# First chunk's gate rows ahead of the others, g copied within SBUF, and the router's third tile as matrix products

## The chip, the core and the metric

One core of one Trainium2 chip runs the whole program. The metric is the device time of one execution in microseconds. The engines named below are PE (TensorE), DVE (VectorE), ACT (ScalarE), POOL (GpSimd) and SP (SyncE, which issues the bulk DMAs).

## The reference

Three layers follow one another. The first is a gated recurrence over 768 steps, for 2 batches of 8 heads of 40 features. With a running maximum m it keeps a 40x40 state C and a vector n:

```python
m_new = np.maximum(f_gate[:, :, t] + m, i_gate[:, :, t])
f_stab = np.exp(f_gate[:, :, t] + m - m_new)
i_stab = np.exp(i_gate[:, :, t] - m_new)
C = f_stab[:, :, None, None] * C + i_stab[:, :, None, None] * np.einsum('bhd,bhe->bhde', vt, kt)
n = f_stab[:, :, None] * n + i_stab[:, :, None] * kt
h_tilde = np.einsum('bhde,bhe->bhd', C, qt)
denom = np.maximum(np.abs(nq), 1.0)          # nq = n . q
y[:, :, t] = o * h_tilde / denom             # o = sigmoid(o_gate)
```

The result is 1536 tokens x 320. The second layer is a dense mixture of 4 experts (320 to 1024, relu, back to 320), weighted by given probabilities. The third chooses one of 8 experts for each token by the largest logit of `x @ w_gate`, gives each expert a capacity of 384 tokens in their order, and scales the result by the chosen probability.

## The kernel before

**Chunks and units.** The 768 steps are cut into 6 chunks of 128. A unit is one chunk of one batch (8 heads); the 12 units run in the order chunk by chunk, batch 0 then 1, so units 0 and 1 are the first chunk. Within a chunk the recurrence is a masked product: scores q.k times a decay matrix, times v. What came before the chunk enters through the state (`state`, 120 x 3 x 123, three groups of heads).

**Gate rows.** On 16 partitions (batch x head) DVE makes, over all 768 steps: `m_run` (scan), `decay`, `g_sum` (a scan of the log decays that restarts in each chunk), its split into two parts `g_split`, the bias rows `rows3[0:16]`, and the arguments `warg`, `garg`, `c_arg`; ACT takes their exponentials. `g_split` is written to DRAM (`g_saved_rows`) by SP and read back as two rows of `g_rows`; PE multiplies them by `spread_w`, which spreads g over 128 partitions and adds the causal mask (`spread_g`). PE transposes `rows3` chunk by chunk (`gate_columns`) and makes the carry factors `c_all`; DVE copies them into `cols3`, the per-step biases and weights.

**A unit** on PE (`attend`): scores (L469, 8 products), first half of `spread_g` for the next unit (L454), the part from before the chunk (L482), the update of the state (L490), the transpose of a finished tile (L508), then the sums with v (L500) in two halves, the second half of `spread_g` between them. ACT (`decays`, L752) makes the decay matrix of the next unit, POOL cuts its corner (`mask`, L926), weighs v (`weigh_v`, L936), scales the state (`carry_state`, L943), adds the new part (`new_state`, L952) and multiplies the output gate by the reciprocal of the denominator (`scale_o`, L964, result `osc`). DVE makes the product `pmat` (L1104), `before` (L1114), `state_new` (L1120), `total` (L1132), the denominator (L1140 to L1144) and `x_tok` (L1149).

**Order.** Each engine runs its own program, in the order in which it is written; they meet only at semaphores (`wait_ge`). `keep_warm` is products without use, to keep PE at work: 44 before the first transposes, 14 in two places. Each unit's data (q and k pairs, q rows, k and v) comes in four loads of SP into one of 4 buffers.

**First expert layer.** For each of 4 experts there are 4 blocks of 384 tokens. A block is `up` (8 tiles f of the hidden layer, 8 products each, L536 to L539) and `down` (3 tiles n of tokens, 24 products each, L551 to L553). ACT and DVE split the hidden tile in a high and a low part (L792, L1198). With the last expert (c = 0 to 3), the router runs beside it, one block behind: for the three tiles of the block before, DVE makes 24 dot products of a token tile with a gate column (`dots`, L1299), two after each of the 8 hidden tiles and 8 more at the end; then `choose_expert` gives `one_hot`, PE counts earlier tokens (`count_earlier`, L608, ahead of tile n = 2), and `gates_of` and `slots_of` give each token's gate and slot. The last group's logits are made on PE (`transpose_y`, L589, `logits`, L599).

## Time and profile before

| | |
|---|---|
| median of 3 runs | 608.98 us (607.63 to 617.74) |
| the profiled execution | 610.95 us |
| its span in the trace | 609.2 us |
| PE busy | 577.8 us, 95% |
| DVE busy | 318.7 us, 52% |
| ACT busy | 213.0 us, 35% |
| POOL busy | 204.2 us, 34% |
| mean granted clock of PE | 0.979 |

The span is what the trace covers; the execution's time is 1.75 us longer. Busy shares are means over a program of several stages; the chain of waits says which engine was last in each.

### The profile page before, as it was taken

Reading aid. Unit: us, or ns where it says so; the run is one execution under the profiler, and the core shown is the slowest. Engines: PE = TensorE matmul, PEld = TensorE weight load, DVE = VectorE, ACT = ScalarE, POOL = GpSimd, SP = SyncE. Lnnn points to the kernel's source line nnn. Section 1 sums busy time; section 2 is a strip of 40 time slices with the busy share of each in tenths; the row PEclk is TensorE's granted clock in tenths of the full one; section 3 lists DMA queues with packets and bytes.
Section 4 is the critical chain, followed back from the end, with each engine's and each line's share of the span. In section 5 each row is a group of like instructions: output and inputs, shape, how many; then the busy total and the mean of one; then the engine's idle time right before and its main releaser. Section 6 shows DMA issues by size and latency. Waiting matters only on the chain.

```text
span 609.2 us, 10906 instructions
## 1 busy us (share of the span) xinstructions
PE 577.8 (95%) x3924; PEld 566.5 (93%) x3924; DVE 318.7 (52%) x741; ACT 213.0 (35%) x457; POOL 204.2 (34%) x226
## 2 busy tenths in 40 slices
PE   3999999999999999999999999999879998899996
PEld 3899989999999999999999999898868998899996
DVE  8389883322332332233233237797844499855472
ACT  5455572311321231232133023023115386546341
POOL 6266556101100110110111022223132467765461
PEclk9699999999999999999999999999987999899999
DMA  6486707941101101110110110111133657764400
GB/s 200 114 261 182 225 30 268 366 179 47 47 1 47 47 0 47 47 46 2 47 47 0 47 48 10 66 61 41 48 122 112 206 182 247 244 223 140 139 16 18
DMA packets 22574, 64.32 MB, mean 106 GB/s; under 512 B 3206, under 2 KB 12559, under 8 KB 22412
## 3 DMA queue, kind: packets, MB, share of 16 engines
q1 hardware_dynamic: 20620, 59.80, 30.0%
q0 software_dynamic: 1920, 4.07, 1.8%
q8 instruction: 21, 0.34, 0.2%
q14 instruction: 13, 0.11, 0.1%
HBM read 52.98 MB, written 13.11 MB: 108 GB/s over the span
## 4 chain that ended last, share of the span: by engine, by line
PE 79%; DVE 10%; ACT 3%; DMA 3%; issue 2%; POOL 2%; POOLq 0%; SPq 0%; DVEq 0%; ACTq 0%
PE bank L536 26%; PE bank L551 8%; PE bank L553 8%; PE bank L552 8%; DVE products L1299 5%; PE bank L539 4%; PE bank L538 4%; PE bank L683 3%; PE bank L682 3%; PE bank L500 3%; PE bank L681 3%; PE bank L469 2%; PE bank L454 1%; PE bank L482 1%; DVE h_lo L1198 1%
## 5 line engine op out<-in xcount | busy, mean ns | idle before, releaser
L792 ACT ACTIVATE h_hi<-bank 128x384 fp32r<-128x384 f32 x192 | 94.5, 492 | 300.6 <-PE bank L539 299.5
L1198 DVE SCALAR_TENSOR_TENSOR h_lo<-bank,h_hi 128x384 fp32r<-128x384 f32 x192 | 105.8, 556 | 111.5 <-ACT h_hi L792 110.6
L906 POOL TENSOR_TENSOR w_lo_odd<-stage,w_hi_odd 128x512 fp32r<-128x512 f32 x24 | 31.3, 1302 | 149.0 <-DVE w_hi_odd L1163 119.7
L906 POOL TENSOR_TENSOR w_lo_even<-stage,w_hi_even 128x512 fp32r<-128x512 f32 x24 | 32.2, 1344 | 118.0 <-DVE w_hi_even L1163 104.8
L536 PE MATMUL bank<-xt_hi,w_hi_even 128*128 (+2 forms) x192 | 65.3, 340 | 3.8 <-DVE h_lo L1198 2.1
L536 PE MATMUL bank<-xt_hi,w_hi_odd 128*128 128x384 f32 (+2 forms) x192 | 62.9, 327 | 2.7 <-DVE h_lo L1198 2.3
L536 PE MATMUL bank<-xt_lo,w_hi_even 128*128 (+2 forms) x192 | 63.7, 332 | 0.0
L536 PE MATMUL bank<-xt_hi,w_lo_even 128*128 (+2 forms) x192 | 63.6, 331 | 0.0
L1207 DVE SCALAR_TENSOR_TENSOR acc<-bank,prob,acc 128x320 f32 (+1 forms) x36 | 19.6, 551 | 80.9 <-PE bank L553 79.8
L536 PE MATMUL bank<-xt_lo,w_hi_odd 128*128 128x384 f32 (+2 forms) x192 | 61.8, 322 | 0.0
L536 PE MATMUL bank<-xt_hi,w_lo_odd 128*128 128x384 f32 (+2 forms) x192 | 61.8, 322 | 0.0
L551 PE MATMUL bank<-w_hi_odd,h_hi 128*128 128x320 f32 x192 | 60.2, 313 | 1.3 <-DVE h_lo L1198 1.3
L551 PE MATMUL bank<-w_hi_even,h_hi 128*128 128x320 f32 x192 | 59.4, 310 | 0.1
L552 PE MATMUL bank<-w_lo_odd,h_hi 128*128 128x320 f32 x192 | 59.4, 309 | 0.0
L553 PE MATMUL bank<-w_hi_even,h_lo 128*128 128x320 f32 x192 | 59.4, 309 | 0.0
L553 PE MATMUL bank<-w_hi_odd,h_lo 128*128 128x320 f32 x192 | 59.3, 309 | 0.0
L552 PE MATMUL bank<-w_lo_even,h_hi 128*128 128x320 f32 x192 | 59.3, 309 | 0.0
L536 PEld LDWEIGHTS bank<-xt_hi,w_hi_even 128*128 128x128 f32 x192 | 36.9, 192 | 4.8 <-DVE h_lo L1198 2.6
L536 PEld LDWEIGHTS bank<-xt_hi,w_hi_odd 128*128 128x128 f32 x192 | 36.1, 188 | 4.2 <-DVE h_lo L1198 4.2
L1299 DVE SCALAR_TENSOR_TENSOR products<-acc,wg_rows 128x320 f32<-128x320 f32 x72 | 38.6, 582 | 0.1
L551 PEld LDWEIGHTS bank<-w_hi_odd,h_hi 128*128 128x128 f32 x192 | 36.1, 188 | 2.1 <-DVE h_lo L1198 2.1
L536 PEld LDWEIGHTS bank<-xt_lo,w_hi_even 128*128 128x128 f32 x192 | 36.9, 192 | 0.0
(187 smaller groups left out, 1347.5 us busy)
## 6 DMA issues: line engine op xcount, KB each, us to landing
stage<-w_moe SPq DMA_DIRECT2D x48, 704.0 KB, 4.1
slot_rows<-empty_row SPq DMA_DIRECT2D x1, 4632.0 KB, 22.8
x_slot<-slot_rows SPq DMA_DIRECT2D x24, 193.0 KB, 4.4
kv<-kv_tok SPq DMA_DIRECT2D x12, 324.0 KB
qk_pair<-qk_pair_t SPq DMA_DIRECT2D x24, 160.0 KB
q_rows<-q_t SPq DMA_DIRECT2D x12, 180.0 KB
sig<-o_tok SPq DMA_DIRECT2D x2, 960.0 KB, 6.3
out<-empty_row SPq DMA_DIRECT2D x2, 960.0 KB, 18.8
```

Of the source, the lines that this page charges most:

```text
L500: mm = pe.matmul(ps_in[:, h * V1:(h + 1) * V1], pmat[:, h, :], v41[j][:, h, :], start=True, stop=True)
L536: pe.matmul(dst, wk[w][:, k, cols], xk(k), start=(n == 0), stop=False)
L538: pe.matmul(dst, w1_hi[w][:, 2, cols], xh(2), start=False, stop=False)
L539: pe.matmul(dst, w1_hi[w][:, 2, cols], xl(2), start=False, stop=True).then_inc(h_psum, 1)
L551: pe.matmul(ps_y[n][:, 0:X], h_hi[:, f, rows], w2_hi[w][:, f, :], start=(f == 0), stop=False)
L552: pe.matmul(ps_y[n][:, 0:X], h_hi[:, f, rows], w2_lo[w][:, f, :], start=False, stop=False)
L553: mm = pe.matmul(ps_y[n][:, 0:X], h_lo[:, f, rows], w2_hi[w][:, f, :], start=False, stop=(f == FT - 1))
L792: act.activation(h_hi[:, f, :], ps_h[f % 3][:, 0:BLOCK], ACT.Relu).then_inc(h_hi_done, 1)
L906: return pool.tensor_tensor(w1_lo[w][:, :, cols], raw1[:, 0:2, :], w1_hi[w][:, 0:2, cols].bitcast(F32), ALU.subtract)
L1198: dve.scalar_tensor_tensor(h_lo[:, f, :], ps_h[f % 3][:, 0:BLOCK], 0.0, h_hi[:, f, :].bitcast(F32), ALU.max, ALU.subtract).then_inc(h_done, 1)
L1207: op = dve.scalar_tensor_tensor(acc[:, tile, 0:X], ps_y[n][:, 0:X], share, acc[:, tile, 0:X], ALU.mult, ALU.add)
L1299: dve.scalar_tensor_tensor(products[k % 3][:], acc[:, t, 0:X], 1.0, wg_rows[:, n % E2, :], ALU.mult, ALU.mult, accum_out=logit[:, t, n % E ...
```

## The change

**Gate rows in two parts.** DVE first makes all rows of chunk 0 (128 steps), then those of the other five. The bias rows of the later chunks come after unit 0, their `garg` and `warg` are made on POOL, their columns are transposed after units 0 and 1 have begun (`bias_columns`, `other_columns`).
**g.** `g_split` is copied straight to `g_rows` within SBUF, one DMA for each of its two parts (two a unit); the DRAM copy is gone. The mask of the second `g_rows` buffer is copied by ACT from the first instead of being made on POOL.
**ACT.** A sigmoid of one column comes first; both large sigmoids stay ahead of the first exp, of 16x128 instead of 16x768; those of the later chunks come after both units' decays.
**No state work in units 0 and 1.** No product with the empty state, no `before`, no `carry_state` and `new_state`; the update is written straight into the state.
**PE.** 110 `keep_warm` products from the moment `ones` is set; then the scores of unit 0 before its first `spread_g`; 24 in unit 0, 12 in unit 1.
**POOL.** `scale_o` of the unit before comes ahead of `weigh_v` and `carry_state`, not behind them.
**Loads.** q rows, k and v are one array, padded to 128 rows; q and k pairs are padded to 48 rows: three loads a unit. SP's loop over units is written out. The first piece of the weights is loaded after all units' data, with the others. `probs` is loaded later and normalised on DVE after the loop of units.
**Router.** Dots for two of three tiles: those of a block's first tile in the same block's `down` phase, those of the second one by one in the next `up` phase. The third tile's logits are made on PE in that phase (transposes ahead of f = 1, products ahead of f = 2). `count_earlier` moves ahead of n = 1, f = 4.

```diff
-    WARM_SHORT, WARM_GAP, WARM_LONG = 44, 14, 34
+    DOT_TILES = 2
+    PE_TILES = [NT * c + DOT_TILES for c in range(BLOCKS1 - 1)] + list(range(TILES - NT, TILES))
+    WARM_SHORT, WARM_GAP, WARM_LONG = 110, (24, 12), 34
...
-                sp.dma_start(q_rows[j][:], q_t[u]).then_inc(unit_in[j], 16)
-                sp.dma_start(kv[j][:], kv_tok[u]).then_inc(unit_in[j], 16)
+                    sp.dma_start(qk_pair[j][s * HALF:s * HALF + QK], qk_pair_t[u, s]).then_inc(unit_in[j], 16)
...
-                sp.dma_start(g_rows[b][0:2].bitcast(F32), g_dram[:, b * HEADS:(b + 1) * HEADS, bass.ts(c, P)]).then_inc(g_in[b], 16)
+                for n in range(2):
+                    sp.dma_start(g_rows[b][n:n + 1].bitcast(F32), g_split[b * HEADS:(b + 1) * HEADS, n, c * P:(c + 1) * P].bitcast(F32)).then_inc(g_in[b], 16)
...
+            load_unit(0, 0)
+            sp.wait_ge(mask_rows, BATCHES)
+            sp.wait_ge(g_lo_done, 1)
+            for b in range(BATCHES):
+                load_g(0, b)
+            load_unit(0, 1)
+            load_unit(0, 2)
+            sp.wait_ge(g_lo_done, 2)
+            sp.wait_ge(g_spread, 2)
+            load_g(1, 0)
+            load_unit(0, 3)
+            sp.wait_ge(g_spread, 4)
+            load_g(1, 1)
             sp.dma_start(prob[:], probs).then_inc(small_in, 16)
             sp.dma_start(wg[:], w_gate).then_inc(small_in, 16)
-            load_unit(0, 0)
...
+            def first_columns():
+                pe.wait_ge(gate_exp, 1)
+                pe.transpose(ps_upd[:, 0:80], rows3[:, 0:P], ident[0:80, 0:80]).then_inc(cols_pe, 1)
...
+            def bias_columns():
+                pe.wait_ge(gate_step, GATE_BIAS)
...
+            def other_columns():
+                pe.wait_ge(gate_exp, 3)
...
+            def attend(i, r, last_chunk=False, opening=None):
...
+                if opening is None:
+                    scores(i, r)
+                if not last and opening != 1:
                     spread_g(i, r + 1, 0)
-                pe.wait_ge(state_done, u + 1)
...
+                if opening == 1:
+                    scores(i, r)
+                    carry_columns()
+                if opening == 1:
+                    pe.wait_ge(state_done, 1)
+                if opening is None:
+                    pe.wait_ge(state_done, u - EMPTY + 1)
...
+                if opening is not None:
+                    keep_warm(WARM_GAP[opening], ones[:], ones[:])
+                if opening == 1:
+                    bias_columns()
...
+            pe.wait_ge(pool_const, CONST_ONES)
+            keep_warm(WARM_SHORT, ones[:], ones[:])
+            pe.wait_ge(pool_const, CONST_SPREAD)
+            scores(0, 0)
             spread_g(0, 0, 0)
+            first_columns()
             spread_g(0, 0, 1)
-            keep_warm(WARM_GAP, ones[:], tri[:])
-            gate_columns()
-            attend(0, 0, warm=WARM_GAP)
-            attend(0, 1)
+            attend(0, 0, opening=0)
...
+                    if c and f == 2:
+                        logits(PE_TILES[c - 1])
+                    if c and f == 1:
+                        transpose_y(PE_TILES[c - 1])
                 def before_products(n, f):
-                    if c and n == 2 and f == 0:
+                    if c and n == 1 and f == 4:
...
+            act.wait_ge(mask_rows, 1)
+            act.activation(g_rows[1][:], g_rows[0][:].bitcast(F32), ACT.Copy).then_inc(mask_rows, 1)
...
-            act.wait_ge(gate_step, GATE_ROWS)
-            act.activation(rows3[32:48, :], warg[:], ACT.Exp).then_inc(gate_exp, 1)
-            act.activation(rows3[64:80, :], garg[:], ACT.Exp).then_inc(gate_exp, 1)
-            act.activation(c_scale[:], c_arg[:], ACT.Exp).then_inc(gate_exp, 1)
+            act.wait_ge(gate_step, GATE_COLS)
+            act.activation(rows3[32:48, 0:P], warg[:, 0:P], ACT.Exp).then_inc(gate_exp, 1)
...
+            act.wait_ge(gate_step, GATE_C)
+            act.activation(c_scale[:], c_arg[:], ACT.Exp).then_inc(carry_exp, 1)
+            act.wait_ge(warg_done, 1)
+            for to, argument in ((32, warg), (64, garg)):
+                act.activation(rows3[to:to + BH, P:], argument[:, P:], ACT.Exp).then_inc(gate_exp, 1)
+            act.wait_ge(bias_done, 1)
...
+            pool.wait_ge(cols_done, 1)
+            weigh_v(0)
+            mask(0)
+            pool.wait_ge(gate_step, GATE_G)
+            pool.tensor_tensor(later_chunks, g_sum[:, later].rearrange("h (c t) -> h c t", t=P),
+                               d_start[:, 1:].unsqueeze(2).broadcast_to([BH, CHUNKS - 1, P]), ALU.add)
+            weigh_v(1)
+            mask(1)
+            pool.wait_ge(gate_step, GATE_BIAS)
+            pool.tensor_tensor(warg[:, later].rearrange("h (c t) -> h c t", t=P), rows3[0:BH, later].rearrange("h (c t) -> h c t", t=P),
+                               g_sum[:].rearrange("h (c t) -> h c t", t=P)[:, 1:, P - 1:P].broadcast_to([BH, CHUNKS - 1, P]),
+                               ALU.add).then_inc(warg_done, 1)
+            for u in range(1, UNITS - BATCHES):
+                scale_o(u - 1)
                 if u + 1 < UNITS - BATCHES:
+                    if u == 1:
+                        pool.wait_ge(cols_done, 2)
+                        pool.wait_ge(carry_done, 1)
                     weigh_v(u + 1)
                     carry_state(u + 1)
-                if u:
-                    scale_o(u - 1)
                 mask(u + 1)
-                new_state(u)
+                if u >= EMPTY:
+                    new_state(u)
...
+            running_max(early)
+            decay_rows(early)
+            chain(dve.tensor_tensor_scan(g_sum[:, 1:P], reset[:, 1:P], decay[:, 1:P], 0.0, ALU.mult, ALU.add))
+            g_parts(early)
+            chain(dve.tensor_tensor(rows3[0:BH, early], gate_i[:, early], m_run[:, 1:P + 1], ALU.subtract))
+            bias_rows(early)
+            chain(dve.tensor_tensor(warg[:, early], rows3[0:BH, early], g_sum[:, P - 1:P].broadcast_to([BH, P]), ALU.add))
+            assert done[0] == GATE_COLS
+            running_max(later)
+            decay_rows(later)
+            chain(dve.tensor_tensor(rows3[0:BH, later], gate_i[:, later], m_run[:, P + 1:S + 1], ALU.subtract))
+            assert done[0] == GATE_ROWS
+            dve.wait_ge(cols_pe, 1)
+            dve.tensor_copy(cols3[:, 0, :], ps_upd[:, 0:80]).then_inc(cols_done, 1)
             chain(dve.tensor_copy(d_start[:].unsqueeze(2), chunks(decay[:])[:, :, 0:1]))
+            chain(dve.memset(chunks(decay[:])[:, 1:, 0:1], 0.0))
+            chain(dve.tensor_tensor_scan(g_sum[:, later], reset[:, later], decay[:, later], 0.0, ALU.mult, ALU.add))
+            assert done[0] == GATE_G
+            chain(dve.tensor_tensor(c_arg[:].unsqueeze(2), chunks(g_sum[:])[:, :, P - 1:P], d_start[:].unsqueeze(2), ALU.add))
+            assert done[0] == GATE_C
...
+            g_parts(later)
+            dve.wait_ge(pool_const, CONSTS)
+            probabilities(0, 0)
+            combine(0, 0)
+            bias_rows(later)
+            assert done[0] == GATE_BIAS
+            probabilities(0, 1)
+            dve.wait_ge(carry_pe, 1)
+            dve.wait_ge(bias_pe, 1)
+            dve.tensor_copy(c_all[:].rearrange("p n c -> p (n c)"), ps_first[0:GR, 0:BATCHES * 3 * CHUNKS]).then_inc(carry_done, 1)
+            dve.tensor_copy(cols3[:, 1:, 0:BH], ps_first[:, P + BH:P + CHUNKS * BH].rearrange("p (c g) -> p c g", g=BH)).then_inc(bias_done, 1)
+            combine(0, 1)
+            dve.wait_ge(cols_pe, 2)
+            dve.tensor_copy(cols3[:, 1:, 2 * BH:], ps_t[:, 80:CHUNKS * 80].rearrange("p (c g) -> p c g", g=80)[:, :, 2 * BH:]).then_inc(cols_done, 1)
+            dve.wait_ge(cols_done, 2)
+            with dve.Fori(0, UNITS // 4 - 1) as i:
+                for r in range(2, 6):
+                    attend(i, r)
...
+                    dve.wait_ge(log_ready, group + 1)
+                    log = ps_log(t.start, t.stop)
                     if group < LAST1:
-                        dve.wait_ge(dot_done, NT * E2 * (group + 1))
+                        t2 = PE_TILES[group]
                         log = logit[:, t, :]
-                    else:
-                        dve.wait_ge(log_ready, group - LAST1 + 1)
...
+            def dots(t, experts):
+                dve.wait_ge(y_free, 3 + 3 * (G1 - BLOCKS1) + t + 1)
+                for one in experts:
+                    k = DOTS * (t // NT) + t % NT * E2 + one
                     if k >= 3:
                         dve.wait_ge(dot_done, k - 2)
-                    dve.scalar_tensor_tensor(products[k % 3][:], acc[:, t, 0:X], 1.0, wg_rows[:, n % E2, :], ALU.mult, ALU.mult,
-                                             accum_out=logit[:, t, n % E2:n % E2 + 1]).then_inc(dot_done, 1)
...
                     if c:
-                        dots(c - 1, f)
+                        dots(NT * (c - 1) + 1, [f])
...
+                    if c < LAST1 and n < 2:
+                        dots(NT * c, range(n * E2 // 2, (n + 1) * E2 // 2))
```

The places where order matters. PE, from its start to the first sums of unit 0, before (`rows` is `rows3`):

```order
L415 MATMUL bank<-tri,ones 128x128 x43
L437 MATMUL bank<-ident,rows 128x16 x5
L454 MATMUL bank<-g_rows,spread_w 128x512 [waits g_in0]
L454 MATMUL bank<-g_rows,spread_w 128x512
L415 MATMUL bank<-tri,ones 128x128 x14
L421 MATMUL bank<-ident,rows 128x80 [waits gate_exp]
L425 MATMUL bank<-c_scale,c_select 120x6 [waits select_done]
L469 MATMUL bank<-qk_pair 128x128 [waits unit_in0]
L415 MATMUL bank<-tri,ones 128x128 x14
L454 MATMUL bank<-g_rows,spread_w 128x512 [waits exp_done,cols_done,g_in1]
L482 MATMUL bank<-state,q_rows 128x123 [waits comb_done,state_done]
L500 MATMUL bank<-kv,pmat 128x41 [waits p_done]
```

and with the change:

```order
L426 MATMUL bank<-ones 128x128 x109
L482 MATMUL bank<-qk_pair 128x128 [waits unit_in0,pool_const]
L471 MATMUL bank<-g_rows,spread_w 128x512 [waits g_in0]
L431 MATMUL bank<-ident,rows 128x80 [waits gate_exp]
L471 MATMUL bank<-g_rows,spread_w 128x512
L471 MATMUL bank<-g_rows,spread_w 128x512 [waits g_in1]
L516 MATMUL bank<-vw,kvq 120x123 [waits vw_done]
L426 MATMUL bank<-ones 128x128 x24
L530 MATMUL bank<-kvq,pmat 128x41 [waits p_done]
```

The scores of unit 0 and its first spread now stand ahead of any transposed column, a single transpose stands ahead of the first sums instead of twelve and the carry products, and the product with `state` is gone.

DVE, from the gates' arrival to the first `pmat`, before:

```order
L1066 SCALAR_TENSOR_TENSOR m_run<-gate_f,gate_i 16x768 [waits gates_in]
L1067 TENSOR_TENSOR decay<-gate_f,m_run 16x768 [waits gate_step]
L1068 TENSOR_TENSOR decay<-decay,m_run 16x768 [waits gate_step]
L1071 SCALAR_TENSOR_TENSOR g_sum<-reset,decay 16x768 [waits gate_step]
L1072 CAST g_split<-g_sum 16x768 [waits gate_step]
L1074 TENSOR_TENSOR g_split<-g_sum,g_split 16x768 [waits gate_step]
L1078 TENSOR_TENSOR rows<-decay,g_sum 16x768 [waits pool_const,gate_step]
L1082 TENSOR_TENSOR gate_f<-rows,g_sum 16x768 [waits gate_step]
L1083 TENSOR_TENSOR gate_i<-g_sum,d_start 16x768
L1089 COPY cols<-bank 128x6x48 [waits gate_pe]
L1091 COPY c_all<-bank 120x36 [waits gate_pe]
L1104 TENSOR_TENSOR pmat<-bank,dmat 128x4x128 [waits s_ready,masked,y_free]
```

and with the change:

```order
L1128 SCALAR_TENSOR_TENSOR m_run<-gate_f,gate_i 16x128 [waits gates_in,gate_step]
L1156 SCALAR_TENSOR_TENSOR g_sum<-reset,decay 16x127 [waits gate_step]
L1137 CAST g_split<-g_sum 16x128 [waits gate_step]
L1138 TENSOR_TENSOR g_split<-g_sum,g_split 16x128 [waits gate_step]
L1160 TENSOR_TENSOR gate_f<-rows,g_sum 16x128 [waits gate_step]
L1128 SCALAR_TENSOR_TENSOR m_run<-gate_f,m_run,gate_i 16x640 [waits gate_step]
L1130 TENSOR_TENSOR decay<-gate_f,m_run 16x640 [waits gate_step]
L1165 TENSOR_TENSOR rows<-gate_i,m_run 16x640 [waits gate_step]
L1168 COPY cols<-bank 128x80 [waits cols_pe,gate_step]
L1171 SCALAR_TENSOR_TENSOR g_sum<-reset,decay 16x640 [waits gate_step]
L1137 CAST g_split<-g_sum 16x640 [waits gate_step]
L1186 TENSOR_TENSOR pmat<-bank,dmat 128x4x128 [waits s_ready,masked,pool_const]
```

The split of g for chunk 0 (`g_split` 16x128) now comes fourth and fifth here; the scan and split of the other chunks stand between the first columns and the first `pmat`.

POOL in the loop of units, one unit, before:

```order
L936 TENSOR_TENSOR vw<-kv,cols 128x328 [waits upd_ready,unit_in3]
L943 TENSOR_TENSOR state_kept<-state,c_all 120x369 [waits state_done]
L964 TENSOR_TENSOR osc<-sig,rden 128x320 [waits x_main,rden_done]
L926 AFFINE_SELECT dmat<-dmat 2x8x2 [waits exp_done]
L952 TENSOR_TENSOR state<-state_new,state_kept 120x369 [waits state_step,state_carried]
```

and with the change:

```order
L1010 TENSOR_TENSOR osc<-sig,rden 128x320 [waits x_main,rden_done,sig_done]
L986 TENSOR_TENSOR vw<-kvq,cols 128x328 [waits upd_ready,unit_in0]
L993 TENSOR_TENSOR state_kept<-state,c_all 120x369 [waits state_done]
L976 AFFINE_SELECT dmat<-dmat 2x8x2 [waits exp_done]
L1002 TENSOR_TENSOR state<-state_new,state_kept 120x369 [waits state_step,state_carried]
```

`osc` (scale_o) moved from behind `vw` and `state_kept` to ahead of them; both now follow its wait for `rden_done`.

## Rows read from the trace of the kernel before

**Rows 1.** The chain that ended last, first 60 us, in order of time: start, us, what.

```profile
3.24 1.76 DVE m_run L1066
...
5.02 0.96 DVE decay L1067
...
6.98 0.19 DVE d_start L1069
...
12.33 2.23 DMA g_saved_rows<-g_split
...
14.57 1.71 DMA g_rows<-g_saved_rows
...
19.28 2.50 PE bank L425 x12
21.77 2.01 PE bank L469 x16
...
34.84 1.09 PE bank L469 x16
...
36.99 0.67 PE bank L490 x6
37.66 0.33 PE bank L508 x3
37.99 0.82 PE bank L500 x8
...
39.93 1.09 PE bank L469 x16
```
**Rows 2.** A window of 1 us on PE: length, busy time, granted clock, DMA share, GB/s.

```profile
26.00:27.00 1.00, 1.00 (x7) 0.50 0.00 0
```
**Rows 3.** Timeline of all engines, first 20 us: start, us, engine, line, operation.

```profile
5.04 1.08 POOL L885 TENSOR_SCALAR_AFFINE_SELECT spread_w<-spread_w 128x128 fp32r<-128x128 f32 x1
...
9.39 4.82 PE L415 MATMUL bank<-tri,ones 128*128 128x128 bf16 x44 [9.39 <-DVE g_sum L1071]
9.69 1.81 ACT L735 ACTIVATE sig<-sig 128x1920 f32<-128x1920 f32 x1 [0.98 <-DMA sig<-o_tok]
...
11.51 1.28 ACT L737 ACT_TABLE_LOAD   x1
...
16.22 0.84 ACT L737 ACTIVATE rows<-gate_f 16x768 f32<-16x768 f32 x1 [3.43 <-DVE c_arg L1084]
...
18.07 2.09 ACT L752 ACTIVATE dmat<-bank,cols 128x128 f32<-128x128 f32 x8
```
**Rows 4.** Timeline of all engines, 20 to 42 us.

```profile
23.91 1.29 DVE L1104 TENSOR_TENSOR pmat<-bank,dmat 128x512 f32<-128x512 f32 x2 [0.27 <-PE bank L469]
...
37.11 0.79 POOL L943 TENSOR_TENSOR state_kept<-state,c_all 120x369 f32<-120x369 f32 x1
37.17 0.76 DVE L1140 SCALAR_TENSOR_TENSOR den<-total 128x8 f32<-128x8 f32 x1
...
38.45 0.72 POOL L964 TENSOR_TENSOR osc<-sig,rden 128x320 f32<-128x320 f32 x1 [0.56 <-DVE rden L1144]
...
40.46 0.23 POOL L926 TENSOR_SCALAR_AFFINE_SELECT dmat<-dmat 2x16 f32<-2x16 f32 x1 [1.28 <-ACT dmat L752]
```
**Rows 5.** The chain again, starts of three blocks of the first expert layer.

```profile
346.37 1.04 PE bank L536 x6
...
368.02 1.04 PE bank L536 x6
...
392.14 1.04 PE bank L536 x6
```
**Rows 6.** Timeline of PE where it waits for the router's choice.

```profile
388.29 0.17 PE L608 MATMUL bank<-one_hot,tri 128*128 128x24 bf16 x1 [1.06 <-DVE one_hot L1252]
```
**Rows 7.** Timeline of PE, the router's logit products of one tile.

```profile
440.75 0.82 PE L599 MATMUL bank<-wg,yT 128*128 128x8 f32 x6
```
**Rows 8.** The page's costliest groups, the router's dot products.

```profile
L1299 DVE SCALAR_TENSOR_TENSOR products<-acc,wg_rows 128x320 f32<-128x320 f32 x72 | 38.6, 582 | 0.1
```

319 lines of the change are left out of this document (156 added, 163 removed).

## The prediction

> **What bounds the kernel now.** I read the page first: PE is busy 95% of the span, so outside a few places only less PE work could help. The chain of waits shows those places. Until 18 us it holds almost no matmul: it is the gate rows on DVE (a scan of 16x768, 1.76 us, two additions of 0.96), then g to DRAM (2.23) and back (1.71) [rows 1]. Then it is all PE, but at half pace: the scores of unit 0 take 2.01 us, those of unit 2, 1.09 [rows 1], and the granted clock still stands at 0.50, the 1.2 GHz level, at 26 [rows 2]. Unit 2 begins at 34.84, unit 3 at 39.93: a unit costs 5.09 us, all on PE [rows 1]. The third place is the last layer of the first expert set. A block begins at 346.37, the next at 368.02: 21.65 us with nothing to wait for. The next takes 24.12 (to 392.14) [rows 5], because DVE is behind with the router's dots and PE waits for its choice [rows 6].
>
> **The opening, step by step.** My ruler is when unit 3 begins on PE, 39.93 now; what follows is paced by PE at 5.09 a unit.
>
> DVE. A fixed part of about 0.15 us (the 16x6 copy took 0.19) plus length: 16x128 costs about 0.42 as scan and 0.28 as addition, 16x640 1.5 and 0.82, a tile 328 to 369 wide 0.5 [rows 1]. The early chain is two scans, two additions, the split of g (two operations), two additions for the bias and one for warg: 3.24 + 1.85 + 0.3, so g of chunk 0 is ready at about 5.4 instead of 12.3, and the early arguments at about 6.3.
>
> The copy of g. One DMA step instead of two removes about 2.2 [rows 1]. But it is queued behind both o_gate halves and unit 0, 2.9 MB; I expect it to land at 11.5 to 12.5, so of the 6.9 us that DVE gains here only some 4 count.
>
> ACT. It must still do both sigmoids before the first exp: the second starts at 9.69 and takes 1.81, then the table load 11.51 + 1.28 = 12.79 [rows 3]. The new dummy sigmoid only takes a table load out of ACT's idle time. The mask copy (128x1024, about 1 us by the sigmoid's 1.81 for 1920 [rows 3]) lies in the idle time ahead of the first sigmoid, which waits for its data: free, unless the mask is late, when it delays the sigmoids by as much. Exp of 16x128 is about 0.3 (16x768: 0.84 [rows 3]): 13.1. Transpose and copy: 13.7. Eight exps, 2.1 to 2.3 [rows 3]: unit 0's decays are complete at 16.0, its mask at 16.2. So ACT, not g, is what the first unit now follows.
>
> DVE again. After the copy at 13.7 it does d_start, the scan of 16x640, c_arg and the split of later g: 0.2 + 0.1 + 1.5 + 0.2 + 1.7 gives 17.4; POOL's garg, 1.4 us by POOL's 369-wide product of 0.79 [rows 4], can lock it out in this stretch, so I take 17.9. Here DVE, not ACT, is late. Product of unit 0 (1.29 [rows 4]) to 19.2, against 25.2 now. Then the state copy, 0.5, while PE does the sums (two times 0.82 in the chain, the second half after the product, with a spread of g [rows 1]), and the copy of the total, 0.5: 20.6; bias rows 0.8: 21.4; product of unit 1 to 22.7. Then it waits for PE: scores 1.1, carry columns 1.25, upd 0.67, twelve warming products 0.65, five small transposes 0.45 at full clock, from 20.2: 24.3. At half clock the same is 2.0 + 2.5 + 1.3 + 1.3 + 0.9, that is 28.2 (2.01 and 2.50 are shown, 1.09 and 0.67 too [rows 1]; the warming by 109 ns each [rows 3]; the rest halved or doubled).
>
> From there, full clock: two copies 0.5, denominator 0.7, state copy 0.5, x of unit 0 behind POOL's scale_o 1.3, total 0.4, last columns 0.4: 28.1 with no overlap, 27.6 with. POOL follows with weigh_v 0.73, carry_state 0.79 and the mask 0.23: 29.4. Product of unit 2 to 30.7, PE's second half 0.7: unit 3 begins at 31.4. Gain 8.5 us at full clock throughout; at half clock the step above costs 3.9: 4.6. Left out of units 0 and 1 are six products of state and the adding; they lie in this sum as zero, since PE is no longer what is last there.
>
> **Which clock.** The 44 warming products before took 4.82 us, 109 ns each [rows 3], and 16 units of scores half as long at 34.84 as at 21.77. So PE ran at the low level at first, whatever the page grants there; the clock rose, fell after PE had little to do between 14.2, when the products end, and 16.3, when g landed, and was low at 26 still, through small transposes and 6-column products. Afterwards PE starts at 1.1 instead of 9.4: 110 products end between 9 (clock up early) and 13 (never up), and scores wait for unit 0 at about 11.5. There will be a hole of up to 2.5 us and again small work. I take two chances in three that part of the opening runs low, and the middle: 6.5 us. The Trainium skill (TensorE: Matmul & The Clock Gate, What's actually happening) says the low clock is the default and activity releases it; by that alone the long run of products would leave the opening at full clock, 8.5 us. The rows of before, where 4.8 us of products did not carry through, speak for less.
>
> **The loop of units.** POOL now does scale_o(u-1) ahead of weigh_v and carry_state. In unit 2 osc starts at 38.45, since it waits for the reciprocals; 0.72 and then two products of at most 0.79 and the mask's 0.23 end at 40.98; today the mask ends at 40.69 [rows 4]. But the product of unit 3 also needs unit 3's scores, which end at 39.93 + 1.09 = 41.02 [rows 1]. It just fits. The denominator, 0.76 us beside POOL's carry_state [rows 4], can only get quicker; x's product may get slower. Zero, bounds -0.5 and +2. The normalising of probs, four small operations, 1.4 us, moves from a hole into the last pass of DVE: 0 to 0.7. Piece 0 of the weights is now loaded with the other three, behind all units; those are not waited for today, and all four are 2.9 MB, under 10 us at the rate at which the first 2.9 MB came (by 12 us): hidden. The unit's loads are 3 instead of 4 and 9% larger; hidden.
>
> **The router.** Per block PE loses 24.12 - 21.65 = 2.47 us [rows 5]. A third of the dots (24 of 72, 38.6 / 72 = 0.54 us each [rows 8]) leaves DVE and another third moves into the down phase before; DVE's choice comes about 2.7 us after the up phase, PE asks for it 5.3 after. So the waits go. PE gets three transposes, 0.33 [rows 1], and a tile's logit products, 0.75 of the 0.82 shown [rows 7], and keeps the count, 0.2: 1.3 us. Gain 1.15 in two blocks; the last gains 1.3, as a wait of 0.5 for the slots of the earlier group stays. Sum 3.6, bounds 2.5 and 4.5.
>
> **Sum.** 6.5 + 3.6 = 10.1 us. The profiled execution took 610.95: 600.9. The median of the runs is 2.0 lower, 608.98: I forecast **599**, 1.6% faster. 2%, about what a measurement of this kernel can tell from no change, would be 596.8.
>
> **Rivals.** (a) *Clock up and short waits*: full gain of 8.5 or a little more, with 3.6 to 4.5: 594.5 to 596.8. For it: DVE's later work may not meet POOL's. Chance 0.25. (b) *Half clock through both first units*: 4.6 or less, 601 to 603. For it: PE's work there is small transposes and products. Chance 0.16. (c) *The change doesn't shorten the opening*: the copy of g is stuck behind the bulk loads, or the mask copy pushes the sigmoids back; unit 0 starts at 16 rather than 13.7, and only 3 to 4 of the opening's gain with the router's remain: 602 to 605. Against it: the queue was nearly empty at 12 us. Chance 0.05. (d) *Slower, by POOL and DVE shutting each other out in the loop*. A POOL select started beside a DVE addition took 1.08, ending with it [rows 1, 3]. If scale_o, weigh_v, carry_state and the mask were each held up so, by some 0.8 us of an addition's 0.96, a unit would take 5.09 + 3.2; over 9 units +29, 628. It makes the kernel slower than before from 10 / 9 = 1.1 us a unit on, by over 2% from 2.5. Against it: the same POOL operations took 0.72 and 0.79 beside DVE work [rows 4]. Chance 0.03. The Trainium skill (SBUF — State Buffer, the section on the engine and DMA ports) has this as a lock held for a whole instruction, between POOL and a DVE operation that reads two SBUF inputs. By that rule x's product (total times osc) would wait for all of weigh_v, 0.7 us; I have this as absorbed by the slack behind the total.
>
> **How the numbers follow.** Forecast, part of the opening at low clock: 597 to 601, chance 0.51. With (a) to (d) that is one. The range leaves out (d) and the far ends of (a) and (c): 594.5 to 604. Faster by over 2%: (a), 0.25. Within 2%: 0.72. Slower: (d), 0.03.
>
> **What would show it.** Right: g_rows lands near 12, first decay near 13.7, product of unit 0 near 18, unit 3's scores at 31 to 35, units at 5.09; blocks of the router at 22.9. Wrong: PE waiting for POOL in the loop; first exp after 14; unit 3 after 36; PE waiting for transposes of the third tile.

## The result and the profile after

The changed kernel took 616.6 us (median of 4, 611.3 to 618.9), the kernel before 609.8 beside it: ratio 1.0124, 95% interval 1.0069 to 1.0179. A second series, 12 runs of the changed kernel beside 17 of the kernel before on one chip, gave 614.5 against 610.7, ratio 1.0070 (1.0026 to 1.0114). A ratio compares the runs within 1.5% of the fastest of their kernel; medians and ranges are of all runs. So it is slower by about 1%, within 2% of the kernel before, and 599 with the range to 604 was wrong. The profiled execution below took 611.34, the shortest of the four (span 609.6, mean granted clock 0.971; the other three 0.957 to 0.963; before: 610.95, 609.2, 0.979).

The chain that ended last, of the changed kernel, in order of time (start, us, what), answers to [rows 1] and [rows 5]:

```profile
4.11 10.00 DMA kvq<-kvq_tok
...
14.24 2.08 PE bank L482 x16
...
17.28 0.24 DVE cols L1168
...
17.75 1.95 DVE g_sum L1171
...
20.63 1.48 issue
22.11 0.68 DVE pmat L1186
...
30.73 3.57 PE bank L530 x16
...
36.04 2.01 PE bank L482 x16
...
43.63 1.09 PE bank L482 x16
...
48.72 1.09 PE bank L482 x16
```
```profile
350.86 1.04 PE bank L572 x6
...
372.50 1.04 PE bank L572 x6
...
395.53 1.04 PE bank L572 x6
...
418.62 1.04 PE bank L572 x6
```

Unit 3 began at 43.63, where [rows 1] has 39.93 and I expected 31.4 to 35.3. Until 14.11 the chain is no longer gate rows but unit 0's own load; from 17.28 to 22.11 it lies on DVE; most of units 1 and 2 runs at half pace (scores of unit 2: 2.01). From 43.63 a unit takes 5.09, as before. The router's blocks start 21.64, 23.03 and 23.09 apart, where [rows 5] has 21.65 and 24.12. Added up from the two profiled executions: 3.7 us lost at unit 3, 0.9 more by the first expert's products (below), 2.9 gained in the router's blocks; that leaves 1.6 at 460 us, of which the last layers give back 1.2.

The clock of TensorE, windows of the two kernels (from:to, length, busy us and count of PE, PEld, DVE, ACT, POOL, granted clock, DMA share, GB/s). Before:

```profile
17.70:27.90 10.20, 10.11 (x65) 9.33 (x64) 3.82 (x9) 3.57 (x14) 3.18 (x5) 0.51 0.51 135
28.00:60.00 32.00, 32.00 (x309) 30.40 (x307) 26.52 (x59) 17.20 (x60) 20.09 (x30) 1.00 0.72 210
```

After:

```profile
0.00:14.00 14.00, 7.59 (x110) 7.42 (x110) 8.55 (x18) 8.78 (x13) 5.00 (x17) 1.00 0.84 245
14.10:20.90 6.80, 6.37 (x37) 5.22 (x38) 3.42 (x7) 3.20 (x12) 1.83 (x3) 0.50 0.85 208
20.90:27.70 6.80, 5.76 (x63) 5.35 (x61) 5.48 (x8) 1.21 (x5) 3.36 (x4) 1.00 0.43 123
27.80:41.40 13.60, 13.60 (x76) 12.37 (x76) 4.87 (x16) 4.91 (x15) 3.76 (x6) 0.50 0.46 124
41.50:60.00 18.50, 18.50 (x183) 17.53 (x181) 15.56 (x34) 10.55 (x36) 12.07 (x18) 1.00 0.60 167
```

The last figure but two of a row is the granted clock: 0.50 is the 1.2 GHz level. (The 1.00 of the first row is too high for its beginning: until 3.86 the warming products took 0.103 us each, 27 in 2.79, and from 3.9 on 0.055, 86 in 4.70.) Before, the low level lasted 10.2 us and was over when unit 1 began. After, it is there for 6.8 us behind a hole of 5.6, gives way for 6.8, and comes back for 13.6, in which PE has no idle time at all: from 27.8 to 41.4 units 1 and 2 are worked at half speed. What stands at the holes, by the timelines of DVE, POOL and PE (start, us, engine, line, operation, idle time before it and what ended it):

```profile
5.75 2.86 SPq L347 DMA_DIRECT2D g_rows<-g_split  x4
...
13.45 0.31 ACT L784 ACTIVATE rows<-gate_f 16x128 f32<-16x128 f32 x1
```
```profile
14.24 2.08 PE L482 MATMUL bank<-qk_pair 40*128 40x128 f32 x16 [5.58 <-DMA kvq<-kvq_tok]
...
22.84 1.08 PE L530 MATMUL bank<-kvq,pmat 128*128 128x41 f32 x8 [1.04 <-DVE pmat L1186]
```
```profile
20.43 1.75 DVE L1138 TENSOR_TENSOR g_split<-g_sum,g_split 16x640 fp32r<-16x640 f32 x1
```
```profile
20.03 1.47 POOL L1020 TENSOR_TENSOR reset<-g_sum,d_start 16x640 f32<-16x640 f32 x1
```

The four copies of g took 0.71 us each to issue on the mean, where a read of g from DRAM before took 0.24 to 0.27; unit 0's data came at 14.11, 0.7 us behind the start of the first exponential; the difference for the later g stood beside POOL's sum, 1.75 instead of the 0.81 it takes alone (below). The normalising of the probabilities now stands in DVE's last pass, and PE waits for it:

```profile
79.71 0.21 DVE psum_p L1285
...
79.94 1.06 DVE psum_p L1287
...
82.35 1.09 PE bank L530 x8
```

### The profile page after: what moved, and what is told of

The parts are those of the page before. It is cut to its first block, busy times and chain, and to the rows that moved or that the text cites. A ratio compares the mean times of both kernels' runs of the same rounds, so it can differ in the third digit from the quotient of the medians.

```text
span 609.6 us, 10961 instructions
## 1 busy us (share of the span) xinstructions
PE 585.8 (96%) x4012; PEld 575.4 (94%) x4012; DVE 306.0 (50%) x702; ACT 214.2 (35%) x465; POOL 200.4 (33%) x221
## 4 chain that ended last, share of the span: by engine, by line
PE 88%; DVE 3%; issue 3%; DMA 3%; ACT 2%; POOL 1%; SPq 1%; POOLq 0%; DVEq 0%; ACTq 0%
PE bank L572 29%; PE bank L587 9%; PE bank L589 9%; PE bank L588 9%; PE bank L575 5%; PE bank L574 5%; PE bank L530 3%; PE bank L727 3%; PE bank L726 3%; PE bank L725 3%; PE bank L482 2%; DMA kvq<-kvq_tok 2%; PE bank L471 1%; PE bank L516 1%; PE bank L508 1%
## 5 line engine op out<-in xcount | busy, mean ns | idle before, releaser
L797 ACT ACTIVATE dmat<-bank,cols 128x128 f32<-128x128 f32 x96 | 27.1, 371 | 29.5 <-PE bank L471 25.7
L572 PEld LDWEIGHTS bank<-xt_hi,w_lo_even 128*128 128x128 f32 x192 | 36.4, 190 | 0.0
```

What stands on the lines that cost most here:

```text
L572: pe.matmul(dst, wk[w][:, k, cols], xk(k), start=(n == 0), stop=False)
L797: op = act.activation(dmat[b][:, h, :], src[:, n * P:(n + 1) * P], ACT.Exp, bias=cols3[:, c, b * HEADS + h:b * HEADS + h + 1])
```

## The experiments

The first run takes half of the change alone. (A span or a mean clock without another name is that of a kernel's profiled execution; medians are of all timed runs.)

**The router alone** (lines of the diff on tiles, dots, transposes, logits and their waits, on the kernel before).

> The kernel before with the router's part of the change alone: six of an expert's dot products of the first two tiles stay on VectorE, the third tile's go to TensorE, and nothing of the opening, the loads or the loop of units is touched. If the blocks of the router gain what the profile of the changed kernel shows (block starts 21.64, 23.03 and 23.09 apart where two of them were 24.12 and 24.18, and the last stretch 0.74 shorter), the run ends 2.9 us below the kernel before, about 607, and the whole loss of the changed kernel stems from its opening. Rival: the router's gain is given back in the stages behind it (its blocks end earlier, but the clock falls for longer there), and this run ends level with the kernel before, within 1 us.

608.6 against 610.9, ratio 0.9955 (0.9917 to 0.9993). The router gains about 2.7 us (0.4 to 5.1 by the interval) and keeps them.

**All but the router.**

> The changed kernel with the router of before: the other half of the change, its opening, loads and loop of units, alone. If the two halves add up, it ends some 3 us above the changed kernel, 619 to 620, or 10 us above the kernel before. Rival: the two halves meet in some other way (the shifted times of the blocks alone bring the clock's falls), and this run is level with the kernel before or with the changed kernel.

616.4, ratio 1.0118 (1.0057 to 1.0180). Some 7 us of loss, where the changed kernel has 4 to 7 with the router's gain in it; by the number it is the rival, level with the changed kernel (616.6) and not the 619 to 620 that the halves add up to, though the intervals don't tell the two apart. The loss is there without the router, and not with the router alone: it is that of the opening, the loads and the loop.

**More products ahead of unit 0.**

```diff
-    WARM_SHORT, WARM_GAP, WARM_LONG = 110, (24, 12), 34
+    WARM_SHORT, WARM_GAP, WARM_LONG = 220, (24, 12), 34
```

> The changed kernel with 220 warming products ahead of unit 0 instead of 110, so that TensorE has no hole of 5.6 us between 8.66 and 14.24. Nothing else is altered, and the data of unit 0 still land at 14.1. Theory of the clock: the fall to 0.50 at 14.2 and what follows it come from the hole, so the clock stays at 1.00 past 14; then unit 3 starts some 4 to 6 us sooner than 43.6, and the run ends 4 to 8 us below the changed kernel, near 610. Rival one: the products of units 0 to 2 wait for data and for VectorE and leave holes of their own, so the clock falls anyway a few us later, and the run gains under 2 us. Rival two: 220 products take longer than until 14.1 (at 0.05 each they end near 14.2) and push unit 0, a loss of up to 1 us.

617.4, ratio 1.0097 (1.0051 to 1.0143): nothing gained. The windows:

```profile
0.00:25.20 25.20, 20.93 (x289) 19.89 (x289) 14.83 (x28) 12.71 (x28) 8.70 (x21) 1.00 0.78 195
25.40:52.50 27.10, 27.10 (x150) 25.13 (x151) 11.57 (x29) 8.20 (x27) 7.74 (x12) 0.50 0.50 135
```

and the timeline of PE:

```profile
15.57 1.31 PE L482 MATMUL bank<-qk_pair 40*128 40x128 f32 x16 [0.29 <-DMA kvq<-kvq_tok]
...
23.04 1.09 PE L530 MATMUL bank<-kvq,pmat 128*128 128x41 f32 x8 [2.20 <-DVE pmat L1186]
...
38.37 2.08 PE L482 MATMUL bank<-qk_pair 40*128 40x128 f32 x16
...
47.94 2.08 PE L482 MATMUL bank<-qk_pair 40*128 40x128 f32 x16
```

The first theory was right up to 14 us and wrong behind: the clock held past unit 0, PE then waited 2.20 us for DVE's product, and 2.4 us later came 27 us of the low level. Units 2 and 3 are 9.57 us apart there, against 5.09: each unit at the low level costs 4.5 us. This is rival one.

**Units 1 and 2 asked for later.**

```diff
             for b in range(BATCHES):
                 load_g(0, b)
+            sp.wait_ge(unit_in[0], UNIT_LOADS)
             load_unit(0, 1)
```

> The changed kernel with one wait more in the load queue: units 1 and 2 are asked for only when unit 0 has landed, so that they no longer share the DMA engines with it. Theory of the data: unit 0's load took 10.0 us since units 1 and 2 ran beside it; alone it lands near 11.5, the hole on TensorE is 2.8 us instead of 5.6, and the first product of probabilities comes no sooner than ACT's first exponential at 13.5 allows; unit 3 starts 2 to 3 us sooner and the run ends 2 to 4 us below the changed kernel, unless unit 1's data, then some 3 us later than now, become the wait (TensorE asks for them at about 26, far behind). Rival: unit 0 lands at 14 all the same, since the output gates' 960 KB and not the later units' data hold the engines; then nothing moves, within 1 us.

```profile
13.66 2.08 PE L483 MATMUL bank<-qk_pair 40*128 40x128 f32 x16 [4.84 <-DMA kvq<-kvq_tok]
```

```profile
11.00:12.00 1.00, 0.00 (x0) 0.00 (x0) 0.00 (x0) 0.98 (x2) 0.00 (x0) 0.50 0.80 287
12.00:12.80 0.80, 0.00 (x0) 0.00 (x0) 0.00 (x0) 0.80 (x1) 0.00 (x0) 0.50 0.06 13
12.80:13.50 0.70, 0.00 (x0) 0.00 (x0) 0.00 (x0) 0.32 (x2) 0.00 (x0) 0.50 0.00 0
```

Unit 0 began at 13.7, and between 13.5 and 15.6 in seven profiled executions of kernels that left those two loads where they were. It lies among them, so no effect of the later units shows; the rival holds: with them out of the way the data came no sooner. Its reason holds only in part. In the run further on with unit 0 ahead of the second half of the gates it landed at 10.1 (issued at 3.11, 7.0 to landing), so its place in the queue counts. But here the DMA engines had all but stopped by 12 and moved nothing from 12.8 to 13.5 (the last two figures of a row), and the load was counted as landed at 13.53 only. What that last microsecond is, no run shows. Its four runs (604.3 to 626.4, clocks 0.941 to 0.982) are too far apart for a ratio; no gain is to be seen.

**DVE in another order:** the scan and split of the later rows ahead of the first columns' copy.

```diff
-            dve.wait_ge(cols_pe, 1)
-            dve.tensor_copy(cols3[:, 0, :], ps_upd[:, 0:80]).then_inc(cols_done, 1)
...
             g_parts(later)
+            dve.wait_ge(cols_pe, 1)
+            dve.tensor_copy(cols3[:, 0, :], ps_upd[:, 0:80]).then_inc(cols_done, 1)
```

> The changed kernel, in which VectorE does the scan of the 640 later rows and its split into two halves ahead of the copy of the first columns, in the hole where it waited from 10.6 to 17.3 for TensorE's transpose. Nothing is left out. Theory of the order on VectorE: in the changed kernel the scan (1.95), its small copies, the cast (0.49) and the difference (1.75, beside GpSimd's sum) stood between the first columns at 17.3 and unit 0's first product with the scores at 22.1; they leave that chain, so that product comes when the mask does, at about 20.3, some 1.8 us sooner, TensorE's hole of 1.04 at 21.8 goes, and the run ends 2 us below the changed kernel where the clock stays as it is, and more where fewer holes keep the clock up (mean granted clock above 0.963). Rival: the clock's fall is not decided by that hole, and the mean clock stays near 0.963; then 0 to 2 us below the changed kernel, about 615.

> The same order on VectorE, and 220 warming products ahead of unit 0, which end with the landing of its data at 14 to 15.3, so that both holes of TensorE's (5.6 us and 1.0 to 2.2 us) are gone. Theory of the holes: with neither hole the clock stays at 1.00 through units 0 and 1, the low stretch of 13.7 to 27.3 us at the loop's entry is not there, the mean clock is at 0.98 or above, and the run ends near 602, 8 us below the kernel before. Rival: the clock falls all the same once the units' small products begin, whatever stands ahead of them, and the run ends at 612 to 617 with a mean clock under 0.97, as with the 220 products alone.

The first, with 110 warming products, took 611.3, ratio 1.0002 (0.9948 to 1.0057), the second, with 220, 609.8, ratio 1.0040 (1.0003 to 1.0076). The order alone brings the changed kernel level with the kernel before, more than the 2 us expected; the second is not the 602 expected, and below its rival's 612 to 617. The timeline of DVE in the second:

```profile
10.96 1.48 DVE L1169 TENSOR_TENSOR_SCAN g_sum<-reset,decay 16x640 f32<-16x640 f32 x1
...
13.17 0.81 DVE L1138 TENSOR_TENSOR g_split<-g_sum,g_split 16x640 fp32r<-16x640 f32 x1
18.00 0.24 DVE L1266 COPY cols<-bank 128x80 f32<-128x80 f32 x1 [4.01 <-PE bank L431]
20.86 1.29 DVE L1184 TENSOR_TENSOR pmat<-bank,dmat 128x512 f32<-128x512 f32 x2 [2.62 <-POOL dmat L976]
```

The product comes 2.9 us behind the columns and no longer 4.8, as forecast, and the split alone takes 0.81. In both profiled executions the low level still came at 31, for 24 us, without a hole above 0.7 us behind the first unit's scores. These two executions were the longest of their kernels (622.2 and 621.8, mean clocks 0.947 and 0.954), so they show that such a fall occurs, and not that it is usual. The strong form of my theory, no hole and no fall, is refuted all the same; the median clock of the runs was 0.966 and 0.976, where the changed kernel has 0.963 over all its 16 runs and the kernel before 0.979.

**Both gaps filled** (220 and 60 products), then **the second alone** (110 and 60).

```diff
-    WARM_SHORT, WARM_GAP, WARM_LONG = 110, (24, 12), 34
+    WARM_SHORT, WARM_GAP, WARM_LONG = 220, (60, 12), 34
```

> The changed kernel with 220 warming products ahead of unit 0 and 60 instead of 24 behind its sums for the state. With the 220 alone the clock held to 25 us and then stood at 0.50 for 27.3 us; the one long hole before the fall was 2.2 us at 20.8. Here it is filled with 36 products of 0.06 us, at no cost while the clock is up. Theory of the holes: the low stretch of 27 us goes, and the run ends some 8 to 12 us below 617, near 606. Rival: the fall comes without the hole, at about the same time; then the run ends at 617 or above it, up to 2 us more since the added products take 0.107 each at the low clock.

> The changed kernel with 60 instead of 24 warming products behind unit 0's sums, and its 110 ahead of unit 0 as they were: the gap of 1.0 to 2.2 us at 21 is filled, that of 5.6 us ahead of unit 0 stays. With both filled the run took 607.9, with the first alone 617.4. If the fall at 14 costs only its own stretch and the second gap is what throws the loop's entry into the low clock, this run ends at 609 to 612, near the one with both filled. Rival: the first hole has already brought the clock down when the 36 added products come, they take 0.107 each (3.9 us, of which 1.0 us in the gap), and what follows is low all the same: 617 to 620.

Both: 607.9, ratio 0.9995 (0.9948 to 1.0042), median clock 0.979. The second alone: 615.0, ratio 1.0125 (1.0072 to 1.0179), median clock 0.964. With the first alone at 1.0097 and neither at 1.0070 to 1.0124, it takes both in most runs. It does not in each: the eight runs with the second alone lie from 605.2 to 618.7, too far apart for their ratio to carry much, seven of them with mean clocks of 0.959 to 0.971, like the changed kernel's (614.5 beside them). The eighth, its profiled execution, took 605.2 at 0.981: the hole ahead of unit 0 was 6.6 us there, the clock low for 10.2 us across it, and back at 1.00 from 21 to 440. The kernel with both lost its clock elsewhere in the profiled execution; its timeline of PE and windows:

```profile
37.31 1.16 PE L482 MATMUL bank<-qk_pair 40*128 40x128 f32 x16
...
76.11 1.08 PE L530 MATMUL bank<-kvq,pmat 128*128 128x41 f32 x8 [0.61 <-DVE pmat L1186]
```
```profile
0.00:78.40 78.40, 75.17 (x834) 71.09 (x836) 58.92 (x132) 42.71 (x130) 40.36 (x66) 1.00 0.72 207
78.80:88.80 10.00, 10.00 (x50) 9.68 (x47) 7.59 (x19) 6.86 (x13) 4.12 (x5) 0.51 0.00 0
```

Unit 3 at 37.31, with the clock at 1.00 all the way there, and a fall 2 us behind the wait for the probabilities.

**Dense products at the loop's entry** (`keep_warm(48, ones[:], ones[:])` behind the last spread before the loop).

> The changed kernel with 48 dense products more between unit 1 and the loop of units; the holes of the opening are all there. They cost 2.7 us at full clock and 5.1 us at half. Theory that the loop's own products are what keeps the clock low once it is entered low (the changed kernel stood at 0.50 for 13.7 us with TensorE without a hole): dense products at its entry bring the clock back before the loop, the low stretch from 27.7 is 6.8 to 10.2 us, and the mean clock rises from 0.963 to 0.97 or more; the run ends level with the changed kernel or up to 3 us below. Rival: what the clock does there depends on the opening's holes alone and not on what stands at the loop's entry; then the products' own time comes on top, 3 to 5 us above the changed kernel, at 620.

619.0, ratio 1.0153 (1.0055 to 1.0251), with 17 us of the low level at 25.6 in its profiled execution, across the added products: the rival. Here they only took time.

**The normalising back in a hole** (with the load of the probabilities right behind unit 0's), on the kernel with both gaps filled, and **all edits together**: new order, normalising, 205 and 32 products.

```diff
             assert done[0] == GATE_ROWS
+            dve.wait_ge(small_in, 32)
+            dve.tensor_reduce(psum_p[:], prob[:], AX_X, ALU.add).then_inc(prob_step, 1)
...
             with dve.Fori(0, UNITS // 4 - 1) as i:
                 for r in range(2, 6):
                     attend(i, r)
-            dve.wait_ge(small_in, 32)
-            dve.tensor_reduce(psum_p[:], prob[:], AX_X, ALU.add).then_inc(prob_step, 1)
```

> The kernel with both gaps filled (220 and 60 warming products), and the normalising of the probabilities moved from the end of the loop of units to VectorE's hole ahead of the first columns. In the run with the gaps filled TensorE waited 0.61 us for it at 75.5, and 2 us behind that the clock stood at 0.50 for 10.2 us; so did it behind the same wait in three other runs. Theory: that wait brings that fall; without it no low stretch stands between 40 and 440, and the run ends 0.8 us of path and up to 5 us of clock below the 607.9 of the kernel with the gaps filled, at 603 to 605. Rival: the fall at 78 comes of something else at the end of the units (their last products wait for nothing else, but the experts' first do, by 0.4 us); it is still there, and the run ends within 1 us of 607.9.

> The changed kernel with four edits at once: the scan of the later rows and its split ahead of the first columns on VectorE, the normalising of the probabilities there too instead of at the end of the loop of units (their load goes into the queue behind unit 0's), 205 warming products ahead of unit 0 and 32 behind its sums. By the theory of the holes none of TensorE's waits before the experts is left but a short one for GpSimd at 19, so the clock stays at 1.00 from the start to the router: unit 3 starts near 35.5 (39.9 before, 43.6 in the changed kernel, 37.3 with the gaps filled alone), the router gives its 2.9, the mean clock is 0.985, and the run ends at 601 to 603, 7 us below the kernel before. Rival: the clock's fall at the loop's entry comes now and then whatever stands ahead of it, and the mean of the runs stays at 0.975 or below and their median within 2 us of the kernel before.

The first: 606.9, ratio 0.9939 (0.9896 to 0.9983), median clock 0.987. It has no low stretch between 40 and 440, but one of 10 us at 29 in the profiled execution. Against 603 to 605 expected, the median is 1.0 below the 607.9 of both gaps filled, which is the rival's bound; against the kernel before beside each it is 0.6% lower, with intervals that overlap. So a gain is likely and its size open. All edits: 606.5, ratio 0.9950 (0.9897 to 1.0003), where 601 to 603 was expected. Its profiled execution (604.6) has the clock at 1.00 throughout the opening, and unit 3 where I expected it for this run (35.5), but 4.5 us behind the 31.4 of the prediction's full-clock sum. Unit 0 begins at 15.47 and not at 11.5: its data landed at 14.1 (issued at 3.89, 10.2 to landing), and the 205 warming products, at 15.5, end later still:

```profile
15.47 1.16 PE L482 MATMUL bank<-qk_pair 40*128 40x128 f32 x16
...
22.97 1.16 PE L482 MATMUL bank<-qk_pair 40*128 40x128 f32 x16
...
30.15 1.16 PE L482 MATMUL bank<-qk_pair 40*128 40x128 f32 x16
...
35.95 1.16 PE L482 MATMUL bank<-qk_pair 40*128 40x128 f32 x16
```
```profile
0.00:440.00 440.00, 434.69 (x3095) 428.17 (x3095) 207.15 (x504) 138.38 (x321) 113.88 (x139) 1.00 0.29 92
```

In the twelve runs the clock was 0.987 or 0.988 in six (601.8 to 604.6) and 0.968 to 0.976 in six (608.5 to 613.5): with the holes gone low runs are fewer than in the changed kernel, where all 16 are at 0.971 or below, but not gone. The rival (mean 0.975 or below, within 2 us of the kernel before) isn't met either: the mean is 0.980, the median 4.8 below.

**Unit 0's load between the output gates' halves**, on the kernel with all edits.

> The first kernel of this batch (all four edits) with unit 0's load put between the two halves of the output gates instead of behind both. Unit 0 then lands near 11 instead of 14 to 15, but the second half of the gates some 3 us later, and ACT does its sigmoid ahead of the first exponential. Theory: the opening is bound twice, by unit 0's data and by ACT's two sigmoids, and the second takes the first's place: the first columns come at 16 to 17.5 as now, and the run ends within 1.5 us of the kernel with the four edits. Rival: data alone were the bound; the first product with the probabilities comes 2 to 3 us sooner, and so does the end.

608.5, ratio 0.9965 (0.9923 to 1.0007). The timeline of ACT:

```profile
15.28 1.80 ACT L783 ACTIVATE sig<-sig 128x1920 f32<-128x1920 f32 x1 [6.12 <-DMA sig<-o_tok]
...
18.39 0.31 ACT L785 ACTIVATE rows<-gate_f 16x128 f32<-16x128 f32 x1
```

PE had its scores at 13.9 and then waited 3.3 us for this exponential, 4.9 later than in the changed kernel. The opening is bound twice, as expected; the columns came later than expected, though, behind 18.39, and the median is 2.0 above the kernel with all edits, where at most 1.5 was expected.

**The old opening, warm, with the new router** (`WARM_SHORT` 176; the router's lines as in the first run).

```diff
-            pe.wait_ge(pool_const, CONSTS)
-            pe.wait_ge(gate_step, GATE_SCAN)
-            keep_warm(WARM_SHORT, ones[:], tri[:])
+            pe.wait_ge(pool_const, 5)
+            keep_warm(WARM_SHORT, ones[:], ones[:])
...
+            pe.wait_ge(pool_const, CONSTS)
+            keep_warm(26, ones[:], ones[:])
             spread_g(0, 0, 0)
```

> The kernel before with the router's part of the change (608.6 where the kernel before took 610.9), and its opening left as it was but for warming products: 176 from the start instead of 44 behind the scan, and 26 more ahead of the first spread of g, where TensorE waited 1.2 to 1.6 us at 14.8 and the clock fell at 17.7 for 10.2 us. Theory of the holes: that fall goes, the columns and unit 0 are worked at full clock (the transposes and sums in 1.8 us instead of 3.6, unit 0's 8.3 us in some 5.5), and the run ends 4 to 5 us below the router's part alone, at 604, with a mean clock of 0.985. Rival: the clock holds no longer here and falls when the units' small products begin, later by as much as the warming lasts; then nothing is gained or up to 4 us lost, as with the changed kernel's 220 products.

606.2, ratio 0.9933 (0.9891 to 0.9976), clock 0.984; 604 was expected. The new router alone had 0.9955 (0.9917 to 0.9993) in another series, so a gain of the warming itself isn't clear of noise. Its profiled execution was its second shortest run (600.2), with the clock at 1.00 until 438. Its timeline of PE:

```profile
20.10 1.16 PE L469 MATMUL bank<-qk_pair 40*128 40x128 f32 x16
...
25.61 1.16 PE L469 MATMUL bank<-qk_pair 40*128 40x128 f32 x16
...
30.38 1.16 PE L469 MATMUL bank<-qk_pair 40*128 40x128 f32 x16
...
35.47 1.16 PE L469 MATMUL bank<-qk_pair 40*128 40x128 f32 x16
```

Unit 3 begins at 35.47, where all edits of the new opening give 35.95. In these two executions the gate rows, the copy of g and the empty state of the first two units bring nothing that the old opening doesn't have at full clock, and the medians, 606.2 and 606.5, agree.

**The changed kernel again**, timed beside the run with the second gap filled.

> The changed kernel itself, beside the kernel above and the same runs of the kernel before. It was timed four times only, at 611.3 to 618.9 with mean clocks of 0.957 to 0.971, and what the clock does in it varies from run to run. Theory: its runs at a mean clock of 0.979 or above, if there are any, lie at 604 to 607, below the kernel before at the same clock (609 to 610), and most runs have a clock under 0.97 and lie at 611 to 619. Rival: the loss is in the path itself; then its runs lie above the kernel before at the same clock too.

Medians are above. None of its 16 runs has a mean clock of 0.979 or more (0.941 to 0.971); of 96 runs of the kernel before in these series, 80 have. Where they meet, at 0.971, three runs of the changed kernel took 610.4 to 611.3 and five of the kernel before 615.1 to 617.6; at 0.968 it is 611.1 against 618.1 to 618.5. So nothing speaks for the rival, a longer path at equal clock. But the mean clock says how much, not where, and it doesn't fix the time: at 0.987 and 0.988 the kernel before took 603.2 to 607.1 in 16 runs and 612.0 to 613.0 in ten. The comparison prices no path, and doesn't refute the rival by itself.

## Why the prediction was wrong

**Which clock** is the step that failed, and with it the start of unit 0. I let the low level cost at most 3.9 us (units 0 and 1) and ended it before unit 2: "I take two chances in three that part of the opening runs low, and the middle". The low level lasted 6.8 + 13.6 us in the profiled execution, 10 + 17 in that of the second series, and reached into unit 2 and, in the second, to 42.6 us. All my cases took what follows unit 2 as paced at 5.09; in the run with 220 products a unit at the low level took 9.57. The mean clock fell from 0.979 to 0.963 (medians), by my estimate 0.016 x 610 = 10 us of TensorE at full clock. No case had units beyond the second at half clock.

How much was the clock and how much the path can be read from the run with both gaps filled, which has the changed kernel's order and the clock at 1.00 until 78 (one profiled execution each, so an estimate). Full-clock forecast 31.4, full clock measured 37.31, changed kernel 43.63: 5.9 us of path and 6.3 of clock. Of the path's 5.9, 3.3 stand at unit 0's first product already (14.8 against 11.5). At full clock the new opening gains 2.6 us over the 39.93 of the kernel before, and not 8.5. So the clock alone doesn't make up the forecast: with both gaps filled the median clock is that of the kernel before, 0.979, and the time only level with it (607.9, ratio 0.9995), still above the range.

The case of a full clock throughout, 8.5 us of gain, did not come: 110 products, then 5.6 us of hole. I had tied it to the Trainium skill's rule (TensorE: Matmul & The Clock Gate, What's actually happening) that activity releases the low clock. The trace agrees at the start, where the warming products went from 0.103 us each to 0.055, and not later: PE was busy from 27.8 to 41.4 without a pause and the clock stayed at 0.50. The measurement decides.

**Unit 0's data**, the other failed step: "scores wait for unit 0 at about 11.5"; it was 14.1, and the hole 5.6 instead of at most 2.5. With the clock up the data landed no sooner, at 14.6 with both gaps filled and 14.1 with all edits. Its load stands behind both halves of the output gates; between them it landed at 10.1. The traffic from 13 to 15 (189 and 194 GB/s) doesn't explain it, since without that of units 1 and 2 unit 0 landed at 13.53 all the same, 0.7 us and more behind the last traffic.

**DVE.** g was ready at 5.7 (5.4 forecast), first exponential at 13.45 (13.1), both near. The wait for unit 0, and its scores at half clock (2.08 us), moved the columns to 17.3 (13.7), and since the DVE work stood behind them in my own list, all of it moved along: product of unit 0 at 22.1 (17.9). The size between was right, 4.8 against 4.2. What I failed to ask is what DVE does while it waits; it was idle for over 6 us ahead of work it could have done.

**ACT and the copy of g.** g was not late (its first product needed no wait at 16.3), but its four issues took 2.86 us of SP and pushed units 1 and 2 back; no product waited for either. Rival (c), unit 0 starting later, happened by another cause than I gave it: its own load, and not g or the mask.

**The loop of units.** POOL's new order cost nothing: 5.09 a unit at full clock in every kernel, so rival (d) is out. (Its example was misread, too: the select ended at 6.12, not with the addition, which ended at 5.98.) The normalising cost 0.9 (unit 3 to the first expert's product behind a wait: 48.3 before, 49.2 after, 48.4 with it moved back), against 0 to 0.7. Behind it the clock fell for 10 us in four of the ten profiled executions that have this wait, and in none of the six without; that was not in the sum. The counts speak for the wait and don't prove it; in the changed kernel's own profiled executions the clock did not fall there.

**The router.** 1.09 a block against 1.15; the last 0.74 instead of 1.3. Sum 2.9 of 3.6 and within its bounds; timed alone, 2.7. Right mechanism, the last block's term mis-sized.

**What stays open.** Why the clock falls at 29 to 31 in some executions of a kernel without holes (none above 0.7 us) and not in others; the router-only kernel, with the old opening, had 13.7 us of it at 42 in its profile too, the longest of its ten runs, at a wait of 1.1 us for g. The filled gaps move the odds; no run here shows what decides. Nor is it known what keeps unit 0's load from counting as landed once the traffic has stopped: its padding to more rows and its larger single array were not tried apart.

## What to carry to other kernels

Where TensorE idles and then meets small products, price the clock first, for every later stage until it is back: here 4.5 us for each unit of 5.09 that the low level covers, where the new opening, even at full clock, gained 2.6 us on the old one as it was. Test the cheap fix on the old code (warming products in its holes) before rewriting it. On an in-order engine, put work that is ready ahead of a wait whose end you don't control.
